# Transposes of two token tiles placed beside the sum of the partial logits, the third beside the transposes of logits and dispatch weights

## The reference

```
x = attention(q, k, v)                  # 2304 tokens x 512
h = x @ w_in                            # 2304 x 2048
g = where(h > 0, h, exp(min(h,0)) - 1)
y = g @ w_out                           # 2304 x 512, x of the next part
logits = y @ phi                        # 2304 x 32 slots
d = exp(logits - logits.max(0)); d /= d.sum(0) + 1e-9     # over tokens
slot_input = d.T @ y                    # 32 x 512
slot_out[e] = relu(slot_input[e] @ w1[e]) @ w2[e]         # 8 experts
c = exp(logits - logits.max(1)); c /= c.sum(1) + 1e-9     # over slots
out = c @ slot_out
```

## Time and profile before

| | |
|---|---|
| median of 3 runs | 915.82 us (915.62 to 916.51) |
| the profiled execution: its own time | 916.68 us |
| its span, first to last instruction | 914.7 us |
| mean granted TensorE clock | 0.996 of full speed |
| TensorE busy | 882.5 us (96% of the span) |
| VectorE, ScalarE, GpSimd busy | 545.9, 470.3, 387.3 us |
| DMA | 76.42 MB, mean 84 GB/s |

### The profile page before, as it was taken

One profiled execution on the slowest core, in us unless ns is written; L12 is line 12 of the kernel. 1 busy time (PEld: TensorE's weight loads), 2 busy tenths in 40 slices (PEclk: granted clock), 3 DMA queues, 4 the chain that ended last, 5 costly groups with the idle time before them and its releaser, 6 DMA issues.

```text
span 914.7 us, 18068 instructions
## 1 busy us (share of the span) xinstructions
PE 882.5 (96%) x7190; PEld 717.9 (78%) x7190; DVE 545.9 (60%) x971; ACT 470.3 (51%) x1017; POOL 387.3 (42%) x269
## 2 busy tenths in 40 slices
PE   4899999999999999998999999999999999999996
PEld 3566676676676766765999999999999999999733
DVE  6878888888888888754654433434433443443423
ACT  3677877878777778686543322232332332322202
POOL 3979999999999999997000000000000000000000
PEclk9999999999999999999999999999999999999999
DMA  6121122222112211303320000200000000476998
GB/s 232 42 77 47 59 79 79 79 79 78 61 71 80 79 40 67 96 1 117 115 70 1 1 1 1 93 1 1 1 1 1 1 1 1 171 243 219 302 374 281
DMA packets 47828, 76.42 MB, mean 84 GB/s; under 512 B 3584, under 2 KB 33408, under 8 KB 47744
## 3 DMA queue, kind: packets, MB, share of 16 engines
q1 hardware_dynamic: 47744, 75.26, 24.5%
HBM read 70.53 MB, written 4.72 MB: 82 GB/s over the span
## 4 chain that ended last, share of the span: by engine, by line
PE 90%; issue 3%; POOL 2%; DVE 2%; ACT 1%; DMA 0%; POOLq 0%; ACTq 0%
PE psum L630 14%; PE psum L694 8%; PE psum L676 7%; PE psum L695 7%; PE psum L677 7%; PE psum L696 7%; PE psum L678 7%; PE psum L609 6%; PE psum L580 5%; PE psum L612 3%; PE psum L614 3%; PE psum L616 3%; POOL acc L1567 2%; PE psum L844 2%; PE psum L821 2%
## 5 line engine op out<-in xcount | busy, mean ns | idle before, releaser
L958 ACT ACTIVATE pt<-psum 128x576 f32<-128x576 f32 x288 | 174.4, 649 | 77.2 <-PE psum L617 76.9
L1196 DVE TENSOR_REDUCE mx<-psum 128x1 f32<-128x512 f32 x256 | 162.4, 678 | 51.4 <-PE psum L580 51.2
L630 PE MATMUL psum<-pt,vs 128*64 128x288 f32 x1152 | 153.6, 412 | 0.0
L1567 POOL TENSOR_TENSOR acc<-acc,pt 128x576 f32<-128x576 f32 x94 | 148.4, 1579 | 0.3 <-ACT pt L958 0.3
L1112 ACT ACTIVATE gf<-psum 128x384 f32<-128x384 f32 x96 | 47.2, 492 | 192.2 <-PE psum L678 191.6
L1400 DVE TENSOR_SCALAR gf<-gf 128x384 f32<-128x384 f32 x96 | 34.6, 360 | 186.7 <-ACT gf L1112 186.7
L694 PE MATMUL psum<-gh,W 128*128 128x384 f32 x384 | 131.5, 342 | 0.0
L695 PE MATMUL psum<-gl,W 128*128 128x384 f32 x384 | 128.4, 334 | 0.0
L696 PE MATMUL psum<-gh,W 128*128 128x384 f32 x384 | 128.4, 334 | 0.0
L676 PE MATMUL psum<-xh,W 128*128 128x384 f32 x384 | 128.4, 334 | 0.0
L678 PE MATMUL psum<-xh,W 128*128 128x384 f32 x384 | 128.4, 334 | 0.0
(11 more groups left out here) (171 smaller groups left out, 2063.8 us busy)
## 6 DMA issues: line engine op xcount, KB each, us to landing
ring<-in_w SPq DMA_DIRECT2D x62, 512.0 KB, 5.7
vs<-in_v SPq DMA_DIRECT2D x16, 576.0 KB, 3.9
kraw<-in_kT SPq DMA_DIRECT2D x15, 576.0 KB, 3.7
qraw<-in_qT SPq DMA_DIRECT2D x15, 576.0 KB, 4.8
out<-ob SPq DMA_DIRECT2D x18, 256.0 KB, 3.3
wst<-in_w_in SPq DMA_DIRECT2D x16, 256.0 KB, 2.8
wst<-in_w_out SPq DMA_DIRECT2D x16, 256.0 KB, 3.0
spare_half<-in_w SPq DMA_DIRECT2D x2, 512.0 KB, 7.4
```

The lines of the kernel that those rows point to most:

```text
L630: ins = mm(psum[64 * s:64 * s + 64, O_BANK, 0:HALF], vs[:, p % NB, s, kt * D:(kt + 1) * D], pt[:, i % NPT, s, :], start=(kt == 0), stop=(k ...
L958: act.activation(pt[:, i % NPT, :, :], t_pair(("T", h, kt))[:, :, 0:HALF], ACT.Exp, scale=SCALE)\
L1196: dve.tensor_reduce(mx[:, b, u // 2, s, u % 2:u % 2 + 1], bank, AX.X, ALU.max).then_inc(s_red, 1)
L1567: pool.tensor_tensor(to, one, other, ALU.add).then_inc(s_acc, 1)
```

## The change

Of the three YTR items of a chunk, two move from step 9 to step 3, behind LT, and the third from step 9 to step 7, behind DTR. ScalarE's copies of them move to the same steps. Nothing is added or removed; the place of LP, LT, LTR, DTR and S stays. There is one place for each chunk c = 1 to 5 (the items belong to chunks 0 to 4; the last chunk's own rows are transposed by other code).

```
-    E_AT = {2: (("LP",),), 3: (("LT",),), 7: (("LTR",), ("DTR",)), 9: (("YTR", 0), ("YTR", 1), ("YTR", 2))}
+    E_AT = {2: (("LP",),), 3: (("LT",), ("YTR", 0), ("YTR", 1)), 7: (("LTR",), ("DTR",), ("YTR", 2))}
     S_AT = 2
...
-                    if f == 9:
-                        for j in range(3):
+                    if f == 3:
+                        for j in range(2):
                             read_rows(c - 1, j)
+                    if f == 7:
+                        read_rows(c - 1, 2)
```

## The result

| | before | with the change |
|---|---|---|
| median | 915.93 us (915.62 to 916.51, 4 runs) | 926.1 us (925.84 to 926.56, 4 runs) |
| ratio | | 1.0112, 95% interval 1.010 to 1.0124 |
| the profiled execution: its own time, its span | 916.68, 914.7 us | 926.11, 924.2 us |
| mean granted TensorE clock | 0.996 | 0.996 |

The change makes the kernel 10.2 us slower. The forecast was 926.0.

What follows compares the result with a forecast made beforehand. TensorE, never idle in the chunks, was taken to bound the kernel. 6.70 + 2.65 + 1.26 - 0.45 = 10.16 us on the median of 915.82 gave 926.0 us, range 924.0 to 929.5.

Steps and rivals of the forecast that it cites:

- Stall A: Step 3, c=2 to 5: YTR 0 waits behind LT for VectorE's running sum, four times, together 6.70 us.
- handover and restart: At nine waits, 0.05 us from VectorE to TensorE plus 0.09 us to start again: 1.26 us in all.
- Stall B: Block H of step 5, c=1 to 5, waits for VectorE's reduce of the logits: 0.53 us each, 2.65 us.
- The restart: TensorE's first matmul after each of nine waits costs 0.09 us extra, bounds 0 and 0.3 us.
- One group less: Transposes join existing groups of small items, saving one change of work per chunk: 0.09 us each, 0.45 us gain.
- upper bound of 12.5 us: Highest sum of the slowdown, with the restart at 0.3 us: 928.3 us.
- ScalarE's copies: Copies of 0.6 us, two in step 3, one in step 7, delay ScalarE's rounding but cost TensorE 0.
- the rival: TensorE's clock falls in the waits for the running sum, 1.6 us each, up to 932.3 us; chance 0.14.
- Only stall A: The wait for the logits' reduce at step 5 doesn't occur: 3.35 us less, 922.6 us; chance 0.04.
- The end: The expert-weight stream sets the end, partly hiding the last chunk's 2.4 us delay: 923.6 us; chance 0.04.
- Not slower: No wait in the chunks is late and one group per chunk is saved: 913.9 to 915.4 us; chance 0.03.

Runs made afterwards that it cites:

- the version that has it alone: The kernel with the change, but only YTR 0 behind LT and YTR 1 and 2 back at step 9: 922.97 us, ratio 1.0072.
- the one that takes it away with the running sum: The kernel with the change, with VectorE's running sum one step earlier, at step 2: 919.27 us, ratio 1.0035.
- The experiment: The kernel with the change, with two extra VectorE reduces ahead of the running sum in c = 3, 4 and 5: 931.2 us, ratio 1.0178.

## Why the prediction was right

- **What bounds the kernel.** Right: TensorE had no idle time in the chunks, and each stall showed in full at the end. The LT distances grow by 10.46 us, the median by 10.2.
- **Stall A**, forecast at 1.62 to 1.74 us and 0.14 for handover and restart. All four came where the forecast had them and for its reason. Alone it lengthens the distances by 1.76, 1.85, 1.81 and 1.78, forecast 1.76, 1.88, 1.81 and 1.81: 7.22 us against 7.26. Shown by the version that has it alone and by the one that takes it away with the running sum.
- **Stall B**, forecast at 0.53 + 0.14 = 0.67 us, five times, 3.35. Alone, at the change's places of the transposes, it lengthens each distance by 0.65 or 0.66. With the 0.05 us that these places save added back it is 0.70.
- **The restart**, forecast at 0.09 us for each of the nine, was mis-sized both ways: about 0.05 behind stall A, where transposes follow, and 0.13 behind stall B, where a stage follows. In sum that is 0.85 us, forecast 0.81.
- **One group less**, forecast at 0.09 us a chunk, a gain of 0.45. The gain is 0.05 to 0.06 a chunk, 0.27 us in all, and its reason was wrong: with the two tiles at step 4 no group is saved, and the distances are as short. The rows point to YTR 2 joining LTR and DTR. In c = 3 the second matmul of stage2 comes 1.67 us after the last L678 ahead of twelve transposes (before) and 1.22 us ahead of eight (step 4), 0.45 us for four; behind LTR and DTR the same four take 0.39 us (1.42 us instead of 1.03).
- **The sum.** The growth of the distances is 10.46 us, the forecast's sum 10.16. Of the 0.30 us between them, the smaller gain is 0.18; most of the rest is the restarts and stalls A that were some hundredths longer. The median grew by 10.17 us and came out 0.1 us from the forecast. That is partly luck: the terms are not that exact, and runs of one kernel differ by more. The upper bound of 12.5 us leaves out the gain of 0.45 that the lower bound of 8.9 has; with it the bound is 12.05 us, or 927.9.
- **ScalarE's copies.** Forecast: the low part of step 3 ready 5.2 us after block H, and nobody waiting. It ended at 663.44, 5.1 us after, and PE has no wait for it.
- **The two stalls add.** 7.22 + 3.27 = 10.49, and the change has 10.46, as the forecast had it from both hanging on the end of a block H of their own.
- **The rivals.** The clock did not fall: 1.00 over the whole stretch. The experiment shows that the rival was near, since 1.2 us more idle time was enough in one of three cases. The fall there cost 1.35 us, forecast 1.6. The rule of the Trainium skill (TensorE: Matmul & The Clock Gate, "A second HAM failure mode: psum-queue depth-cycling"), by which short idle times from bank cycling make the clock swing, is not what the nine stalls of the change show, with the granted clock at 1.00. "Only stall A" fell with the waits for L1342 and L1337. The end took up nothing that shows, where that rival had 2.4 us: from the last LT to the end of the span it is 54.0 us, before 54.3, and 53.8 to 54.4 in the versions without a stall. "Not slower" would have needed the running sum 1.7 us earlier; the version that runs it a step earlier, and the reduce too, comes out there, at 915.69.

## What to carry to other kernels

When work of several kinds shares banks in rotation, moving an item doesn't only move its instructions: it changes which reader each of the following items waits for. For an item that is moved, and for the four behind it, look up what frees the bank and when that reader runs; a list of which semaphore each instruction waits for, before and after, shows it in two lines. If a wait turns out late, move the reader: here running two of VectorE's readers a step earlier gave back all 10 us, and placing the transposes a step later did so too.

## What the runs showed of the hardware

- In a stop of TensorE of 2.8 us between dense matmuls the granted clock fell to half in one of three traced cases, within the stop (0.52 over the microsecond in which it ended), and it came back some 3 us later (0.78 in 814 to 815). It cost 1.35 us. It stayed at 1.00 in all traced stops of 1.5 to 1.65 us between these matmuls, four with the change and four with one tile behind LT. In the attention part it fell during the second of two stops of about 1 us.
- After a wait for VectorE, a stage of twelve matmuls took 2.21 us instead of 2.08, so this stop costs 0.13 us beyond its own length, besides the 0.05 to 0.06 us of handover from VectorE. With eight transposes behind the wait it was about 0.05 us. The weights weren't loaded ahead across the wait: in c = 3 the weight load of YTR 0 started at 660.66, 0.05 us after the running sum ended at 660.61:

```profile
660.66 0.86 PEld L734 LDWEIGHTS psum<-ident,yT 128*128 128x128 f32 x8 [2.29 <-DVE s_run L1388]
```
